# The inverse of the softmax sums: from a reciprocal on VectorE to a logarithm and an exponential on ScalarE with one Newton step, and the order of the work around it

## The chip, the cores and the metric

The kernel runs on one core of a Trainium2 chip. The metric is the device time of one execution in microseconds (us), the median over several runs. PE is TensorE (PEld its loading of weights), DVE is VectorE, ACT is ScalarE, POOL is GpSimd, and SP is the engine that issues most of the DMAs.

## What is computed

Three layers follow each other. The first is attention over hashed buckets (batch 2, 8 heads, 768 positions, 64 features a head):

```
mask = q_bucket[:, :, :, None] == k_bucket[:, :, None, :]
scores = scale * np.matmul(q, k.transpose(0, 1, 3, 2))
scores = np.where(mask, scores, -1000000000.0)
scores = scores - np.max(scores, axis=-1, keepdims=True)
attn = np.exp(scores)
attn = attn / (np.sum(attn, axis=-1, keepdims=True) + 1e-09)
return np.matmul(attn, v)
```

Its result, turned to 1536 tokens of 512 features, goes through a dense layer (a product with w_in, a softmax gate, a layer norm, a product with w_out), and that through a mixture of 8 experts in which each token takes one. The change touches the attention alone: there are 16 (batch, head) pairs, and for each of them 768 sums of exponentials, of which the inverse (with 1e-9 added) scales the 768 columns of the output.

## The kernel before

All engines run programs of their own, written out by hand in the order in which they are to run, and semaphores alone tie them together. The 16 heads go through a software pipeline. In the turn of head h, TensorE does six steps (kt = 0 to 5). Each step holds one block of "leading" scores of a head one or two further on (`leading`, L465, two matmuls of queries in rows; only their maxima are wanted) and the transposed scores of head h against one block of 128 keys (`products`, L481, four matmuls, L491 and L492). ScalarE takes the exponentials of those (`weights_of`, L1022, instruction on L1027) into the tile `PT`, and GpSimd adds them up over the six blocks into `acc` (`add`, L1234, instruction on L1242).

Step kt = 2 of head h holds more: TensorE turns the maxima of head h+1 (`turn_maxima`, L476, instruction on L478), multiplies the second half of the weights of head h-1 with V (`values(h-1, (3, 4, 5))`, twelve matmuls on L503), and adds the sums of head h-1 over the partitions with a matrix of ones (`sums`, L507, four matmuls on L512). After step 5 come `values(h, (0, 1, 2))`, and for even h the hashes of a pair of heads two further on (`hashes`, L455).

VectorE takes the maxima of the leading scores, a block at a time (`maximum`, L727, instruction on L730). The leading scores have two places in PSUM: `leading(h, j)` waits on `s_nm` until maximum j-2 of the same count has been read, so TensorE can be at most two blocks ahead of VectorE. `place_maxima` (L740) writes the turned maxima of the next head into a row of its operand. `inverse` (L748) copies the mean row out of PSUM (L751), adds 1e-9 to the sums (L752) and takes the reciprocal in place (L754) in the tile `rec`; `attended` (L756) forms (values + mean) times `rec` in two instructions (L762) and writes the attention's output `xT`. VectorE's order in the turn of head h is: maxima 4 and 5 of head h+1, the gathering of the six (`maxima`, L732), for odd h the bits of the hashes, maximum 0 of h+2, `place_maxima(h+1)`, `inverse(h-1)`, maximum 1 of h+2, `attended(h-1)`, maxima 2 and 3 of h+2.

ScalarE's order in the turn is: the weights of kt = 0, for odd h the high parts of a later pair, the weights of kt = 1, a scaling of dense-layer weights (L1040), the weights of kt = 2, `weights_high(h)` (L1044), the weights of kt = 3, 4 and 5. GpSimd's order is: for odd h the low parts of a later pair (L1231), the first addition of head h, `weights_low(h)` (L1247), the other four additions.

One PSUM bank, `RB`, holds in turn the maxima turned by TensorE, the sums of a head, and the hashes; another, `PVB`, the products with V. The semaphores `s_mc` (maxima placed), `s_rec` (the steps of the inverse), `s_bits` and `s_fin` (a head's output written) say when they are free. After head 15 the same engines go on with the dense layer: TensorE's `hidden` products (L533 to L535), `soft` on VectorE (from L771) and ScalarE (L1050), the taking of the next tokens (L1057 on ScalarE, L1252 on GpSimd).

Of the kernel before, what the change touches and what calls it, by code (L numbers as in the profile page):

```python
# [39 lines left out]
ACT = mybir.ActivationFunctionType  # L40
# [48 lines left out]
C_SLOT = C_LOW + E * E  # L89
C_TOK = C_SLOT + SLOTS  # L90
C_ALT = C_TOK + NT
C_ALL = C_ALT + E - 1


def constants():

    c = np.zeros((P, C_ALL), np.float32)
    c[:, C_ID:C_ID + P] = np.eye(P)


    for group in range(4):
        for head in range(2):
            for n, sign in enumerate((1, -1) if group % 2 == 0 else (-1, 1)):
                r = slice(group * GROUP + head * BITS + n * NBITS, group * GROUP + head * BITS + (n + 1) * NBITS)
                c[r, C_THR] = LEAST if sign > 0 else -ABOVE
                c[r, C_TOP] = -BIG if group % 2 == 0 else 1.0
                if group < 2:
                    c[:, C_SIGN:C_SIGN + P][:, r] = sign
    c[:, C_TRI:C_TRI + P] = np.triu(np.ones((P, P)), 1)
    c[:, C_ONE:C_ONE + P] = 1  # L110
    c[:, C_EXP:C_EXP + E] = np.arange(E) - E
    c[:, C_J:C_J + NT] = np.arange(NT) * P


    c[:, C_J] = -1
    c[:, C_LOW:C_LOW + E * E] = np.tril(np.ones((E, E)), -1).reshape(1, -1)
    c[:, C_SLOT:C_SLOT + SLOTS] = np.arange(SLOTS)
    for n in range(NT):
        c[:, C_TOK + n] = (n % B) * S + (n // B) * P + np.arange(P)
    c[:, C_ALT:C_ALT + E - 1] = (-1.0) ** np.arange(E - 1)  # L120
    return c


# [11 lines left out]
def build(nc, qT, kT, vP, proj_d, w_solu, g_ln, w_gates, w1, w2, cst_d, out):  # L135
    with ExitStack() as ctx:
# [52 lines left out]
        def many(name, word, n, width, dt=F32):  # L189
            return [at(f"{name}{i}", word + i * width, [P, width], dt)[:, :] for i in range(n)], word + n * width  # L190
# [27 lines left out]
        PT = PT.rearrange("p (k g q) -> p k g q", k=KT, g=2)  # L218
        w = (w + 7) // 8 * 8
        acc, w = many("acc", w, 2, S)  # L220
        (rec,), w = many("rec", w, 1, HALF)
        stg, w = many("stg", w, 2, DM)
        empty = at("empty", mid - 2 * DM, [P, ROW])

# [37 lines left out]
        ld_w = [sem(f"ld_w{c}") for c in range(2)]  # L262
        s_high, s_low, s_ws, s_wh, s_wl = sem("s_high"), sem("s_low"), sem("s_ws"), sem("s_wh"), sem("s_wl")
        ld_v = [sem(f"ld_v{c}") for c in range(2)]
        (s_hash, s_bits, s_slot, s_nm, s_mm, s_mt, s_mc, s_st, s_exp, s_acc, s_pv, s_rb, s_rec,
         s_fin, s_ones, s_zeros) = [sem(n) for n in ("s_hash", "s_bits", "s_slot", "s_nm", "s_mm", "s_mt", "s_mc",
                                            "s_st", "s_exp", "s_acc", "s_pv", "s_rb", "s_rec", "s_fin", "s_ones", "s_zeros")]


        m_xh = sem("m_xh")  # L270
# [24 lines left out]
        def wait(eng, s, v):  # L295

            if not isinstance(v, int) or v > 0:
                eng.wait_ge(s, v)
# [71 lines left out]
        def _(sp):  # L370
# [17 lines left out]
                    fill_2(sp, h, n)  # L388

            def load_v(h):  # L390
                wait(sp, s_rb, h - 1)
                sp.dma_start(V[h % 2], vP[h:h + 1].rearrange("o p (k d) -> p (o k) d", k=KT)).then_inc(ld_v[h % 2], 16)

            def load_w(m):
# [57 lines left out]
        def _(pe):  # L452
# [22 lines left out]

            def turn_maxima(h):  # L476
                pe.wait_ge(s_mm, h + 1)
                m = pe.transpose(PS[0:TILES, RB, 0:P], mm_[:, h % 2 * TILES:(h % 2 + 1) * TILES], ident)  # L478
                m.then_inc(s_mt, 1)

# [26 lines left out]
            def sums(h):  # L507

                pe.wait_ge(s_acc, (KT - 1) * (h + 1))
                wait(pe, s_rec, 3 * h - 1)  # L510
                for g in range(2):
                    m = mm(PS[g * D:(g + 1) * D, RB, 0:HALF], cst[:, C_ONE:C_ONE + D],  # L512
                           acc[h % 2][:, g * HALF:(g + 1) * HALF], start=True, stop=True)
                m.then_inc(s_rb, 1)
# [24 lines left out]
            for h in range(HEADS):  # L539
                for kt in range(KT):  # L540
                    ahead = (h + 1, kt + TILES - 2) if kt < 2 else (h + 2, kt - 2)
                    if ahead[0] < HEADS:
                        leading(*ahead)
                    products(h, kt)
                    if kt == 2:
                        if h + 1 < HEADS:
                            wait(pe, s_rec, 3 * h - 4)
                            pe.wait_ge(s_bits, min(PAIRS, 2 + (h + 1) // 2))
                            turn_maxima(h + 1)
                        if h > 0:  # L550
                            values(h - 1, (3, 4, 5))
                            if h + 1 < HEADS:
                                pe.wait_ge(s_mc, h + 2)
                            sums(h - 1)
                values(h, (0, 1, 2))
                if h % 2 == 0 and h // 2 + 2 < PAIRS:
                    wait(pe, s_rec, 3 * h - 1)
                    hashes(h // 2 + 2, RB)
            hidden(0, 0, 0, True)
            values(HEADS - 1, (3, 4, 5))  # L560
            sums(HEADS - 1)
            hidden(0, 0, 1, True)


# [144 lines left out]
        def _(dve):  # L709
# [17 lines left out]
            def maximum(h, j):  # L727
                col = h % 2 * TILES + j
                dve.wait_ge(s_slot, TILES * h + j + 1)
                dve.tensor_reduce(nm[:, col:col + 1], slot(h, j), AX.XY, ALU.max, negate=True).then_inc(s_nm, 1)  # L730
# [16 lines left out]

            def inverse(h):  # L748

                dve.wait_ge(s_rb, h + 1)  # L750
                dve.tensor_copy(mu[:, h % 2:h % 2 + 1], PS[:, PVB, HALF:HALF + 1]).then_inc(s_rec, 1)  # L751
                dve.tensor_scalar(rec, PS[:, RB, 0:HALF], EPS, None, ALU.add).then_inc(s_rec, 1)  # L752
                dve.wait_ge(s_rec, 3 * h + 2)
                dve.reciprocal(rec, rec).then_inc(s_rec, 1)  # L754

            def attended(h):  # L756

                p, c = h // 2, h % 2
                dve.wait_ge(s_rec, 3 * h + 3)
                for g in range(2):  # L760
                    mine = slice(g * D, (g + 1) * D)
                    m = dve.scalar_tensor_tensor(  # L762
                        out=xT[c * D:(c + 1) * D, p * S + g * HALF:p * S + (g + 1) * HALF], in0=PS[mine, PVB, 0:HALF],
                        scalar=mu[mine, c:c + 1], in1=rec[mine, :], op0=ALU.add, op1=ALU.mult)
                m.then_inc(s_fin, 1)

            def soft(n, b, first):
                h2 = PS[:, 2 * b:2 * b + 2, :]
# [33 lines left out]
            for h in range(HEADS):  # L802
                if h + 1 < HEADS:
                    maximum(h + 1, TILES - 2)
                    maximum(h + 1, TILES - 1)
                    maxima(h + 1)
                if h % 2 == 1 and h // 2 + 2 < PAIRS:
                    hash_bits(h // 2 + 2, RB)
                if h + 2 < HEADS:
                    maximum(h + 2, 0)  # L810
                if h + 1 < HEADS:
                    place_maxima(h + 1)
                if h > 0:
                    inverse(h - 1)
                if h + 2 < HEADS:
                    maximum(h + 2, 1)
                if h > 0:
                    attended(h - 1)
                if h + 2 < HEADS:
                    maximum(h + 2, 2)  # L820
                    maximum(h + 2, 3)
# [194 lines left out]
        def _(act):  # L1016
            fn = nc.scalar.activation

            act.dma_start(hashw[:, :], proj_d).then_inc(s_cst, 16)
            act.dma_start(cst[:, :], cst_d).then_inc(s_cst, 16)  # L1020

            def weights_of(h, kt, g):  # L1022
                act.wait_ge(s_st, 2 * (KT * h + kt) + g + 1)
# [5 lines left out]
            def high_parts(p):  # L1029
                act.wait_ge(ld_r[p % 2], 32 * (p // 2) + 32)  # L1030
                if p > 0:
                    for h in (2 * p - 2, 2 * p - 1):
                        ready_1(act, h)
                        ready_2(act, h)
                for r, high in zip(R[p % 2], (Hq, Hk)):
                    fn(high, r, ACT.Copy).then_inc(s_high, 1)

            def weights_scaled(m):
                act.wait_ge(ld_w[m % 2], 16 * (m // 2) + 16)
# [31 lines left out]
            for h in range(HEADS):  # L1071
                weights_of(h, 0, 0)
                weights_of(h, 0, 1)
                if h % 2 == 1 and h // 2 + 2 < PAIRS:
                    high_parts(h // 2 + 2)
                weights_of(h, 1, 0)
                weights_of(h, 1, 1)
                weights_scaled(h)
                weights_of(h, 2, 0)
                weights_of(h, 2, 1)  # L1080
                if h == HEADS - 1:
                    act.wait_ge(s_rows0, 16 * SLOTS)
                weights_high(h)
                for kt in (3, 4, 5):
                    weights_of(h, kt, 0)
                    weights_of(h, kt, 1)
                if h == HEADS - 2:
                    act.wait_ge(s_fin, HEADS // 2)
                    take(0, 0, 0, True)
            soft(0, 0, True)  # L1090
            act.wait_ge(s_fin, HEADS)
            take(1, 1, 0, True)
# [263 lines left out]
```

## Time and profile before

| | |
|---|---|
| time of the kernel before | 713.75 us, median of 3 runs (712.77 to 714.27) |
| the profiled execution | 709.71 us, its span 707.6 us |
| busy in the span | PE 598.6 us (85%), DVE 400.0 (57%), POOL 268.5 (38%), ACT 259.0 (37%) |
| mean granted clock of TensorE | 0.925 |
| attention | from the start to about 287 us of the span |

The busy time of PE is that of pipelined matmuls, of which the ends are modelled, so its share is not a share of its peak. Shares over the whole span mix the three layers; the attention has to be read by itself, one head's turn at a time. Times in the views are microseconds from the start of the span, unless marked ns.

### The profile page before, as it was taken

To read this page: it belongs to the slowest core of one execution; us is meant where nothing else is said; L and a number is where in the kernel's file an instruction comes from. 1 tells how busy PE (TensorE), PEld (TensorE's weight loads), DVE (VectorE), ACT (ScalarE), POOL (GpSimd) and SP (SyncE) were. 2 spreads that over 40 slices of the span, in tenths; PEclk is the share of its full clock that TensorE was granted. 3 is DMA by queue.
4 is the path that set the end of the run, shared out by engine and by line. 5 is a ranking of instruction groups with operands and counts; after the bars stand their busy time and mean duration, and the time that the engine had idled before them with its cause. 6 is when DMAs were issued, how large, how long until landed. Compare 5 with 4: busy or idle time off the path is not lost.

```text
span 707.6 us, 9729 instructions
## 1 busy us (share of the span) xinstructions
PE 598.6 (85%) x2886; PEld 440.4 (62%) x2887; DVE 400.0 (57%) x525; ACT 259.0 (37%) x403; POOL 268.5 (38%) x188
## 2 busy tenths in 40 slices
PE   3879798888988888699999999602999999999994
PEld 1545454554555544588888887402788788778883
DVE  3737777766677752666566566352445554655611
ACT  1334444444444342122222224312444554545410
POOL 4375767676777675223224223462001010010101
PEclk8689999999999999899999999755999999999997
DMA  6778384674827000300000000347517465665500
GB/s 184 171 215 233 80 239 123 176 192 114 206 69 182 27 12 1 119 1 1 0 0 0 0 0 1 119 157 244 209 51 253 157 213 205 196 217 180 148 19 29
DMA packets 39266, 83.90 MB, mean 119 GB/s; under 512 B 7485, under 2 KB 10429, under 8 KB 39232
## 3 DMA queue, kind: packets, MB, share of 16 engines
q1 hardware_dynamic: 31376, 71.04, 34.5%
q10 hardware_dynamic: 5616, 6.12, 3.4%
q0 software_dynamic: 2240, 6.31, 2.3%
q8 instruction: 18, 0.29, 0.2%
q14 instruction: 16, 0.13, 0.1%
HBM read 52.09 MB, written 12.35 MB: 91 GB/s over the span
## 4 chain that ended last, share of the span: by engine, by line
PE 70%; DVE 13%; issue 4%; DMA 3%; ACT 3%; POOL 2%; SPq 2%; ACTq 1%; DVEq 0%; POOLq 0%
PE PS L503 11%; DVE at_rec L754 6%; PE PS L664 5%; PE PS L666 4%; PE PS L665 4%; PE PS L645 4%; PE PS L646 3%; PE PS L647 3%; PE PS L491 3%; PE PS L533 3%; PE PS L535 3%; PE PS L578 3%; PE PS L534 3%; PE PS L472 3%; PE PS L580 3%
## 5 line engine op out<-in xcount | busy, mean ns | idle before, releaser
L1027 ACT ACTIVATE at_PT<-PS 128x384 f32<-128x384 f32 x192 | 84.6, 491 | 135.2 <-PE PS L492 134.3
L730 DVE TENSOR_REDUCE sb_nm<-PS 128x1 f32<-128x768 f32 x96 | 89.2, 947 | 43.7 <-PE PS L472 41.3
L1242 POOL TENSOR_TENSOR at_acc<-at_acc,at_PT 128x768 f32<-128x768 f32 x64 | 107.6, 1681 | 14.8 <-ACT at_PT L1027 10.3
L952 DVE TENSOR_TENSOR at_W<-at_raw,at_W 128x2048 f32 (+1 forms) x30 | 68.0, 2291 | 71.2 <-ACT at_W L1097 68.5
L1318 POOL DMA_INDIRECT out<-at_yb,sb_to x16 | 15.8, 985 | 204.7 <-DVE at_yb L964 204.7
L1097 ACT ACTIVATE at_W<-at_raw 128x2048 f32 (+1 forms) x32 | 60.4, 1911 | 61.7 <-issue 31.1
L503 PE MATMUL PS<-at_PT,at_V 128*64 128x385 f32 x384 | 80.0, 557 | 3.1 <-DVE at_xT L762 2.7
L472 PE MATMUL PS<-at_B,at_A 76*128 76x384 f32 x192 | 58.6, 394 | 28.0 <-DVE sb_nm L730 23.3
L491 PE MATMUL PS<-at_A,at_B 102*128 102x384 f32 x192 | 73.9, 385 | 9.5 <-ACT at_PT L1027 9.5
L472 PEld LDWEIGHTS PS<-at_B,at_A 76*128 76x128 f32 x192 | 34.4, 205 | 54.9 <-DVE sb_nm L730 31.8
L492 PE MATMUL PS<-at_A,at_B 128*128 128x384 f32 x192 | 67.3, 350 | 0.0
L1273 POOL TENSOR_TENSOR at_cn<-at_eb,sb_mv 128x1024 f32<-128x1024 f32 x12 | 22.7, 1894 | 108.5 <-DVE sb_mv L783 108.5
L664 PE MATMUL PS<-at_W,at_hTh 128*128 x128 | 52.1, 407 | 5.1 <-DVE at_hTl L983 4.9
L645 PE MATMUL PS<-at_W,at_xsh 128*128 x128 | 52.1, 407 | 3.2 <-DVE at_xsl L956 3.2
L503 PEld LDWEIGHTS PS<-at_PT,at_V 128*64 128x64 f32 x384 | 29.1, 152 | 40.4 <-issue 34.4
L491 PEld LDWEIGHTS PS<-at_A,at_B 102*128 102x128 f32 x192 | 37.5, 195 | 26.6 <-ACT at_PT L1027 20.4
L666 PE MATMUL PS<-at_W,at_hTl 128*128 x128 | 50.7, 396 | 0.0
L646 PE MATMUL PS<-at_W,at_xsh 128*128 x128 | 50.5, 395 | 0.0
L665 PE MATMUL PS<-at_W,at_hTh 128*128 x128 | 50.5, 395 | 0.0
L647 PE MATMUL PS<-at_W,at_xsl 128*128 x128 | 50.4, 394 | 0.0
L533 PE MATMUL PS<-at_wsp,at_xch 128*128 128x512 f32 x96 | 39.9, 416 | 6.2 <-POOL at_xcl L1252 6.2
L754 DVE RECIPROCAL at_rec<-at_rec 128x384 f32<-128x384 f32 x16 | 40.9, 2553 | 0.5
(154 smaller groups left out, 1101.6 us busy)
## 6 DMA issues: line engine op xcount, KB each, us to landing
at_raw<-w SPq DMA_DIRECT2D x32, 1024.0 KB, 5.9
at_A<-at_H SPq DMA_DIRECT2D x32, 192.0 KB, 2.7
at_B<-at_H SPq DMA_DIRECT2D x28, 192.0 KB, 3.7
rows_by_expert<-at_empty SPq DMA_DIRECT2D x19, 257.0 KB, 5.3
at_XS<-rows_by_expert ACTq DMA_DIRECT2D x17, 256.0 KB, 2.7
at_stg<-w_solu SPq DMA_DIRECT2D x16, 256.0 KB, 4.0
at_V<-vP SPq DMA_DIRECT2D x16, 192.0 KB, 3.8
at_Re<-qT SPq DMA_DIRECT2D x4, 384.0 KB, 5.0
```

The lines of the kernel that those rows point to most:

```text
L472: m = mm(slot(h, j)[:, g, :], A1[t][0:ROWS1, j * P:(j + 1) * P], B1[t][0:ROWS1, g * HALF:(g + 1) * HALF], start=True, stop=True)
L491: mm(PS[:, STB + g, 0:HALF], B1[t][0:ROWS, at_k], A1[t][0:ROWS, at_g], start=True, stop=False)
L503: m = mm(PS[g * D:(g + 1) * D, PVB, 0:HALF + 1], V[h % 2][:, kt, :], PT[:, kt, g, :], start=(kt == 0), stop=(kt == KT - 1))
L645: mm(PS[:, g, :], xsh[:, x_k], W[:, high], start=(k == 0), stop=False)
L646: mm(PS[:, g, :], xsh[:, x_k], W[:, low], start=False, stop=False)
L664: mm(PS[:, 4 + c, :], hTh[:, h_f], W[:, high], start=(f == 0), stop=False)
L665: mm(PS[:, 4 + c, :], hTh[:, h_f], W[:, low], start=False, stop=False)
L666: m = mm(PS[:, 4 + c, :], hTl[:, h_f], W[:, high], start=False, stop=(f == FB - 1))
L730: dve.tensor_reduce(nm[:, col:col + 1], slot(h, j), AX.XY, ALU.max, negate=True).then_inc(s_nm, 1)
L754: dve.reciprocal(rec, rec).then_inc(s_rec, 1)
L1027: fn(PT[:, kt, g, 0:HALF], PS[:, STB + g, 0:HALF], ACT.Exp, scale=SCALE).then_inc(s_exp, 1)
L1242: pool.tensor_tensor(total, PT[:, 0, :, 0:HALF] if kt == 1 else total, PT[:, kt, :, 0:HALF], ALU.add).then_inc(s_acc, 1)
```

## The change

The reciprocal (L754) and the addition of 1e-9 (L752) leave VectorE. ScalarE takes ln(sum + 1e-9) out of PSUM into `rec`, with 1e-9 as a bias from a new constant column, and then exp(-rec) in place. VectorE refines it by one Newton step in two instructions: err = (sum + 1e-9) times rec, then rec = (2 - err) times rec. ScalarE does its part after `weights_high(h)`.

The order changes as well. TensorE does the sums of head h-1 first, then their products with V, and then turns the maxima of head h+1, now once VectorE has read the sums. VectorE does the inverse and `attended(h-1)` directly after maximum 0 of head h+2, then maximum 1, and `place_maxima(h+1)` only after that. The table set that holds both functions is loaded ahead by name. The load of V waits for the products with V in place of the sums.

```diff
+            act.preload_act_table_set("natural_log_exp_and_others")
...
+            def inverse(h):        # ScalarE
+                act.wait_ge(s_rb, h + 1)
+                wait(act, s_fin, h)
+                fn(rec, PS[:, RB, 0:HALF], ACT.Ln, bias=cst[:, C_EPS:C_EPS + 1]).then_inc(s_ln, 1)
+                act.wait_ge(s_ln, 2 * h + 1)
+                fn(rec, rec, ACT.Exp, scale=-1.0).then_inc(s_ln, 1)
...
             def inverse(h):        # VectorE
-                dve.wait_ge(s_rb, h + 1)
-                dve.tensor_copy(mu[:, h % 2:h % 2 + 1], PS[:, PVB, HALF:HALF + 1]).then_inc(s_rec, 1)
-                dve.tensor_scalar(rec, PS[:, RB, 0:HALF], EPS, None, ALU.add).then_inc(s_rec, 1)
-                dve.wait_ge(s_rec, 3 * h + 2)
-                dve.reciprocal(rec, rec).then_inc(s_rec, 1)
+                dve.wait_ge(s_ln, 2 * h + 2)
+                dve.scalar_tensor_tensor(out=err, in0=PS[:, RB, 0:HALF], scalar=EPS, in1=rec,
+                                         op0=ALU.add, op1=ALU.mult).then_inc(s_rec, 1)
+                dve.wait_ge(s_rec, 4 * h + 1)
+                dve.scalar_tensor_tensor(out=rec, in0=err, scalar=2.0, in1=rec, reverse0=True,
+                                         op0=ALU.subtract, op1=ALU.mult).then_inc(s_rec, 1)
...
             def attended(h):
-                dve.wait_ge(s_rec, 3 * h + 3)
+                dve.wait_ge(s_pv, 2 * h + 2)
+                dve.tensor_copy(mu[:, c:c + 1], PS[:, PVB, HALF:HALF + 1]).then_inc(s_rec, 1)
+                dve.wait_ge(s_rec, 4 * h + 3)
...
             def turn_maxima(h):
                 pe.wait_ge(s_mm, h + 1)
+                wait(pe, s_rec, 4 * (h - 1) - 3)
...
             def sums(h):
                 pe.wait_ge(s_acc, (KT - 1) * (h + 1))
-                wait(pe, s_rec, 3 * h - 1)
+                pe.wait_ge(s_bits, min(PAIRS, 2 + h // 2 + 1))
+                pe.wait_ge(s_mc, min(HEADS, h + 2))
...
                     if kt == 2:        # TensorE
+                        if h > 0:
+                            sums(h - 1)
+                            values(h - 1, (3, 4, 5))
                         if h + 1 < HEADS:
-                            wait(pe, s_rec, 3 * h - 4)
-                            pe.wait_ge(s_bits, min(PAIRS, 2 + (h + 1) // 2))
                             turn_maxima(h + 1)
-                        if h > 0:
-                            values(h - 1, (3, 4, 5))
-                            if h + 1 < HEADS:
-                                pe.wait_ge(s_mc, h + 2)
-                            sums(h - 1)
...
             hidden(0, 0, 0, True)
+            sums(HEADS - 1)
             values(HEADS - 1, (3, 4, 5))
-            sums(HEADS - 1)
             hidden(0, 0, 1, True)
...
                     maximum(h + 2, 0)        # VectorE
+                if h > 0:
+                    inverse(h - 1)
+                    attended(h - 1)
+                if h + 2 < HEADS:
+                    maximum(h + 2, 1)
                 if h + 1 < HEADS:
                     place_maxima(h + 1)
-                if h > 0:
-                    inverse(h - 1)
-                if h + 2 < HEADS:
-                    maximum(h + 2, 1)
-                if h > 0:
-                    attended(h - 1)
```

In the diff the three marks "ScalarE", "VectorE" and "TensorE" are added here to tell which engine's program a piece is in.

## Rows read from the trace of the kernel before

**Rows 1.** Chain that ended last, in the turn of head 8: start, us, engine and line

```profile
161.04 0.67 PE PS L512 x4
...
164.94 0.82 DVE sb_nm L730
```

**Rows 2.** Instructions grouped by line, 50 to 300 us: xcount | busy us, mean ns | idle before

```profile
L1027 ACT ACTIVATE at_PT<-PS 128x384 f32<-128x384 f32 x174 | 76.4, 491 | 126.5 <-PE PS L492 126.0
...
L754 DVE RECIPROCAL at_rec<-at_rec 128x384 f32<-128x384 f32 x16 | 40.9, 2553 | 0.5
...
L762 DVE SCALAR_TENSOR_TENSOR at_xT<-PS,sb_mu,at_rec 64x384 f32<-64x384 f32 x32 | 19.6, 613 | 0.5
...
L1044 ACT ACTIVATE at_wsp<-at_stg 128x512 fp32r<-128x512 f32 x14 | 9.1, 648 | 0.0
L752 DVE TENSOR_SCALAR at_rec<-PS 128x384 f32<-128x384 f32 x16 | 8.8, 548 | 0.0
```

**Rows 3.** Timeline, turn of head 8 (even): start us, us, engine line op [idle before]

```profile
158.68 0.27 PE L478 MATMUL PS<-sb_cst,sb_mm 128*6 128x128 f32 x1
...
159.42 0.64 ACT L1044 ACTIVATE at_wsp<-at_stg 128x512 fp32r<-128x512 f32 x1
...
161.38 1.68 POOL L1242 TENSOR_TENSOR at_acc<-at_acc,at_PT 128x768 f32<-128x768 f32 x1
...
161.73 0.16 DVE L751 COPY sb_mu<-PS 128x1 f32<-128x1 f32 x1 [1.76 <-PE PS L512]
...
163.83 0.34 PE L492 MATMUL PS<-at_A,at_B 128*128 128x384 f32 x1
165.81 0.62 PE L472 MATMUL PS<-at_B,at_A 76*128 76x384 f32 x2 [1.64 <-DVE sb_nm L730]
```

**Rows 4.** Timeline, turn of head 9 (odd): PE and POOL

```profile
176.33 0.27 PE L478 MATMUL PS<-sb_cst,sb_mm 128*6 128x128 f32 x1
...
178.01 1.56 POOL L1242 TENSOR_TENSOR at_acc<-at_PT 128x768 f32<-128x768 f32 x1
179.51 1.32 POOL L1247 TENSOR_TENSOR at_wsp<-at_stg,at_wsp 128x512 fp32r<-128x512 f32 x1
180.76 7.18 POOL L1242 TENSOR_TENSOR at_acc<-at_acc,at_PT 128x768 f32<-128x768 f32 x4
```

**Rows 5.** Line 788: duration ns min/median/max; then the timeline around one such instruction

```profile
L788 DVE TENSOR_TENSOR sb_var_all<-sb_var_all,sb_rs x12: 1758/1764/1772, 292.4 to 438.4; 128x1 f32 x8, 128x1 f32<-128x1 f32 x4
...
306.45 1.76 DVE L788 TENSOR_TENSOR sb_var_all<-sb_var_all,sb_rs 128x1 f32<-128x1 f32 x1
...
306.30 1.89 POOL L1273 TENSOR_TENSOR at_cn<-at_eb,sb_mv 128x1024 f32<-128x1024 f32 x1 [10.92 <-DVE sb_mv L783]
308.14 0.61 POOL L1277 COPY at_x<-at_x2b 128x512 f32<-128x512 f32 x1
```

**Rows 6.** Waits of PE (us in total, times, longest), 52 to 250 us

```profile
PE PS L472 <- DVE sb_nm L730: 21.3, 13, 1.6
```

**Rows 7.** Busy time by stretch: PE, PEld, DVE, ACT, POOL, granted clock, DMA share, GB/s

```profile
150.46:153.87 3.41, 3.41 (x12) 2.04 (x13) 2.61 (x4) 0.98 (x2) 3.12 (x3) 0.50 1.02 303
```

**Rows 8.** Timeline of VectorE: the copy that begins the inverse, turns 5, 6 and 7

```profile
116.02 0.16 DVE L751 COPY sb_mu<-PS 128x1 f32<-128x1 f32 x1 [1.80 <-PE PS L512]
...
130.10 0.16 DVE L751 COPY sb_mu<-PS 128x1 f32<-128x1 f32 x1 [1.76 <-PE PS L512]
...
146.09 0.16 DVE L751 COPY sb_mu<-PS 128x1 f32<-128x1 f32 x1 [1.80 <-PE PS L512]
```

**Rows 9.** Timeline from the end of head 15 into the dense layer

```profile
274.25 2.16 PE L503 MATMUL PS<-at_PT,at_V 128*64 128x385 f32 x12 [1.35 <-DVE at_xT L762]
...
284.69 0.39 PE L535 MATMUL PS<-at_wsp,at_xcl 128*128 128x512 f32 x1
...
286.71 1.23 DVE L771 TENSOR_REDUCE sb_nm<-PS 128x1 f32<-128x1024 f32 x1
```

**Rows 10.** Timeline of ScalarE at the start of the span

```profile
1.70 1.28 ACT L1036 ACT_TABLE_LOAD   x1 [1.54 <-PEq L1349]
```

More of the change, by code:

```diff
@@ L91 @@
 C_ALT = C_TOK + NT
-C_ALL = C_ALT + E - 1
+C_EPS = C_ALT + E - 1
+C_ALL = C_EPS + 1
 def constants():
@@ L120, in constants @@
     c[:, C_ALT:C_ALT + E - 1] = (-1.0) ** np.arange(E - 1)
+    c[:, C_EPS] = EPS
     return c
@@ L220, in build @@
         acc, w = many("acc", w, 2, S)
-        (rec,), w = many("rec", w, 1, HALF)
+        (rec, err), w = many("rec", w, 2, HALF)
         stg, w = many("stg", w, 2, DM)
@@ L264, in build @@
         ld_v = [sem(f"ld_v{c}") for c in range(2)]
-        (s_hash, s_bits, s_slot, s_nm, s_mm, s_mt, s_mc, s_st, s_exp, s_acc, s_pv, s_rb, s_rec,
+        (s_hash, s_bits, s_slot, s_nm, s_mm, s_mt, s_mc, s_st, s_exp, s_acc, s_pv, s_rb, s_ln, s_rec,
          s_fin, s_ones, s_zeros) = [sem(n) for n in ("s_hash", "s_bits", "s_slot", "s_nm", "s_mm", "s_mt", "s_mc",
-                                            "s_st", "s_exp", "s_acc", "s_pv", "s_rb", "s_rec", "s_fin", "s_ones", "s_zeros")]
+                                            "s_st", "s_exp", "s_acc", "s_pv", "s_rb", "s_ln", "s_rec", "s_fin", "s_ones", "s_zeros")]
         m_xh = sem("m_xh")
@@ L390, in load_v @@
             def load_v(h):
-                wait(sp, s_rb, h - 1)
+                wait(sp, s_pv, 2 * h - 2)
                 sp.dma_start(V[h % 2], vP[h:h + 1].rearrange("o p (k d) -> p (o k) d", k=KT)).then_inc(ld_v[h % 2], 16)
@@ L545, in _ @@
                     if kt == 2:
+                        if h > 0:
+                            sums(h - 1)
+                            values(h - 1, (3, 4, 5))
                         if h + 1 < HEADS:
-                            wait(pe, s_rec, 3 * h - 4)
-                            pe.wait_ge(s_bits, min(PAIRS, 2 + (h + 1) // 2))
                             turn_maxima(h + 1)
-                        if h > 0:
-                            values(h - 1, (3, 4, 5))
-                            if h + 1 < HEADS:
-                                pe.wait_ge(s_mc, h + 2)
-                            sums(h - 1)
                 values(h, (0, 1, 2))
                 if h % 2 == 0 and h // 2 + 2 < PAIRS:
-                    wait(pe, s_rec, 3 * h - 1)
+                    pe.wait_ge(s_mc, h + 2)
                     hashes(h // 2 + 2, RB)
             hidden(0, 0, 0, True)
+            sums(HEADS - 1)
             values(HEADS - 1, (3, 4, 5))
-            sums(HEADS - 1)
             hidden(0, 0, 1, True)
@@ L764, in attended @@
                         scalar=mu[mine, c:c + 1], in1=rec[mine, :], op0=ALU.add, op1=ALU.mult)
-                m.then_inc(s_fin, 1)
+                    m.then_inc(s_rec if g == 0 else s_fin, 1)
             def soft(n, b, first):
@@ L1083, in _ @@
                 weights_high(h)
+                if h > 0:
+                    inverse(h - 1)
                 for kt in (3, 4, 5):
@@ L1089, in _ @@
                     take(0, 0, 0, True)
+            inverse(HEADS - 1)
             soft(0, 0, True)
```

## The prediction

> **What bounds the kernel now.** I read the chain of waits first, then the timeline of one even and one odd head. The chain of head 8 leaves TensorE after the sums (161.04 + 0.67) and comes back to it through VectorE, of which the last link is maximum 1 of the head two further on, 164.94 to 165.76 [rows 1]. Between lie the copy, the addition of 0.55 and the reciprocal, 16 of them at 2553 ns [rows 2]. The timeline shows the other side: TensorE has its last product of kt = 4 in hand by 163.83 + 0.34, and then sits idle 1.64 us until 165.81, released by the maximum [rows 3]. So in each turn TensorE waits for VectorE, and VectorE had before that waited 1.76 us for the sums. Whatever shortens the way from sums to maximum 1 is on the path, until TensorE's own work ends later.
>
> I set a mark at the start of the turning of the maxima, 158.68 in head 8 and 176.33 in head 9 [rows 3, 4]. The old order has VectorE start at 3.05 after the mark, the maximum end at 7.08 and TensorE go on at 7.13.
>
> **The change, step by step** (us after the mark; the stretch from the mark to kt = 3 is what is reordered).
>
> TensorE: the sums take 0.67 [rows 1]. Turn, products with V and sums together took until 3.05; without the turn (0.27) they end at 2.78. In the chain the sums begin at 2.36 and VectorE sees them at 3.05, 0.7 later; with 0.2 for the filling of the first matmul ScalarE may start at 0.9.
>
> ScalarE: it is busy with `weights_high` until 159.42 + 0.64, that is 1.38, so that and not the sums lets it begin. The trace holds no logarithm. Nearest are the exponential out of PSUM of the same shape, 491 ns, and a copy in SBUF of 512 columns, 648 ns [rows 2]; both new instructions lie between. I take 0.55 for the first (it has a bias by pointer) and 0.52 for the second, each near the row of its own width: 1.38 + 0.55 + 0.02 + 0.52 = 2.47. ScalarE then idles until the weights of kt = 3, so its 1.1 us a turn cost nothing. Without that cover each would delay the next exponentials.
>
> VectorE, first instruction (err): one operand in PSUM and one in SBUF, as L762 (613 ns) and nearly L752 (548). At 0.61 it ends at 2.50 + 0.61 = 3.11. The removed addition and reciprocal, 3.1 us, go; the copy stays and moves.
>
> VectorE, the Newton step: both tensors in SBUF, 384 columns; I take 0.55, bounds 0.5 to 0.61 by the same two rows. Here stands the question of the whole forecast. The one two-operand SBUF instruction of before that starts while GpSimd computes is L788, on one column: it takes 1758 ns at least, in all 12 cases, and at 306.45 + 1.76 ends as GpSimd's instruction does, 306.30 + 1.89. GpSimd's next, which starts at 308.14, did not hold it up further [rows 5]. I read: such an instruction waits for GpSimd's running one, and then goes first. The Trainium skill, "SBUF — State Buffer", section "Who interferes with whom", gives VectorE's second SBUF port and GpSimd's as one shared pair under an exclusive lock. By that rule the Newton step waits just as L788 does, while by its duration alone it would not; the two sums are those of the first and the third case below.
>
> Even turns: at 3.13 GpSimd is inside an addition from 161.38 for 1.68, until 4.38. The step runs 4.38 to 4.93. The copy adds 0.08, `attended` two times 0.613, maximum 1 takes 0.82: 7.06 to 7.1, and TensorE goes on at 7.13, as before. Gain 0.0 in each of six turns (2 to 12). TensorE still waits there, less long: its turn of the maxima waits for err until 3.13 in place of 2.78, so kt = 3 and 4 end 0.3 later, at 5.8, and the wait is 1.35.
>
> Odd turns: the running addition ends at 178.01 + 1.56 = 179.57, or 3.24, and `weights_low` is next, from 179.51 [rows 4]. The step is ready at 3.13, a tenth earlier, and as L788 goes first: 3.24 + 0.55 + 0.08 + 1.23 + 0.82 = 5.92, TensorE at 5.97 in place of 7.13, or 1.16; it is itself not ready before 5.8. I take 1.1, for seven turns (1 to 13; the first is colder, and taken alike): 7.7.
>
> Turns 14 and 15 have no maximum to wait for; there `values(h, ...)` waits 1.35 for `attended` [rows 9]. That now ends at 4.93 + 0.08 + 1.23 = 6.24, and TensorE is ready at about 6.1 to 6.5. Two times 1.1: 2.2.
>
> After head 15 VectorE's `soft` began at 286.71, right behind `attended`. The half of `hidden` that it needs ends at 284.69 + 0.39 whatever the order before it; now that is last, with `attended` some 2.7 earlier. Gain 1.5.
>
> **The clock.** The 13 waits of TensorE for the maximum sum to 21.3 us [rows 6]. Seven times in the same stretch the granted clock falls to 0.50 for 3.4 us, as at 150.46, right behind this wait in the turn of head 7 [rows 7]: the lower of TensorE's two levels, 1.2 against 2.4 GHz. From copy to copy the turns took 14.08 (from 116.02), 15.99 and, with a fall at 150.46, 15.64 to 161.73 [rows 8, 3]: a turn of the first kind with a fall costs 15.64 less 14.08, 1.56, and one of the other kind 1.6 to 1.7. I take 1.6. In the new order no wait reaches 1.64: odd turns 0.35 and 0.2, even turns 0.35 and 1.35 apart from each other. The trace has no wait of 1.35 by which to tell, so the bounds are all seven falls gone, 11.3, and none, 0. I take all gone, since 6 of the 13 waits of 1.64 already passed without one.
>
> Costed at nothing: the table set (one load of 1.28 us at 1.70, before any input has landed [rows 10], now by name); `place_maxima` about 5 us later, at 7.1 to 8.05, wanted only by the next turn's first products, behind three more steps and the products with V; the load of V, released at 2.9 in place of 3.05 and behind it SP's other loads; GpSimd, held up at most 0.6 a turn by the Newton step, with its run ending 11.6 after the mark in a turn of 15 [rows 4].
>
> Sum: 7.7 + 0 + 2.2 + 1.5 + 11.3 = 22.7 from 709.71, the profiled execution's own time (its span 707.6 and 2.1 around it), which is 687.0. That execution lies 4.0 below the median, so against the median it is **691**.
>
> **The rivals.**
> - The Newton step loses to GpSimd's next instruction in odd turns as well and waits until 179.51 + 1.32 (4.5): all 13 turns gain nothing, 2.2 + 1.5 + 11.3 = 15.0, **699**. For it: the margin is 0.1 us, and errors of 0.1 in three durations of ScalarE and VectorE.
> - It is never held (L788 is a tensor-tensor instruction, this a scalar-tensor-tensor one): 13 times 1.1 + 2.2 + 1.5 + 11.3 = 29.3, **684.5**. Against it: L788, 12 times in 12.
> - The falls stay where 1.35 us of waiting stays: **702** with odd turns free, **710** with all held.
> - Slower: held behind GpSimd's whole run. In odd turns `weights_low` and four additions stand back to back until 180.76 + 7.18, or 11.6. If the step had to wait for an empty engine, maximum 1 would come 11.6 less 3.24 later than at 5.92, 14.3, and TensorE lose 7.1 in each of seven turns: 50 less what the ends give back, **750 to 765**. It decides from about 4.5 on, where the held step makes TensorE later than 7.13. Against it: L788 with another GpSimd instruction right behind.
> - Not done as said: a table load before each logarithm and each exponential, two of 1.28 a turn. The path grows by 2.6 and gains 1.1 at most: 15 times 1.5 or more slower, **735 and up**. For it only that the default choice could differ from the named one.
>
> **How the numbers follow.** The first case has 0.38, held in all turns 0.23, never held 0.12, falls that stay 0.16, the two slower ones 0.05 and 0.03, and 0.03 remains for gains eaten by things that I don't see. The range 682 to 705 takes in the first three cases and the milder of the clock's; without the clock's doubt, the likeliest one's own range is 688 to 695. A measurement of this kernel tells 0.2%, 1.4 us, from no change. Faster by more than that: 0.89; within it 0.03; slower 0.08.
>
> **What would show it.** In the changed profile: the reciprocal's line gone; a logarithm and an exponential of about 0.5 us each, starting 1.3 after the sums' start, one table load at the start; err at 0.6; the Newton step long (1.7 to 1.8) in even turns, ending with GpSimd's addition, and 0.6 to 0.7 in odd ones; turns of about 14.1 and 14.9; waits for the maximum below 1.4; a granted clock of 1.00 between 52 and 230 us. Wrong if the step lasts 1.9 or more in odd turns (699), if it is 0.55 everywhere (684.5), if falls are still there, or if the wait of the maxima's turn is much over 0.4, which would say that ScalarE is later than I take it.

## The result and the profile after

The changed kernel takes 692.14 us (median of 4 runs, 691.57 to 694.88) against 713.26 for the one before: a ratio of 0.974, interval 0.970 to 0.978. The profiled execution took 691.57, its span 689.5. The forecast was 691. The number is close; the clock's term of its sum was not, as the sections below show. One execution of a kernel in the experiments ("Maximum 1 ahead of attended", with the reciprocal: 782.3 us at a mean granted clock of 0.741) is left out of its ratio; without it that kernel's median is 669.0 in place of the 669.2 given there.

First the new instructions, grouped by line (mean ns of one is the last number ahead of the second bar):

```profile
L754 DVE SCALAR_TENSOR_TENSOR at_rec<-at_rec,at_rec 128x384 f32<-128x384 f32 x16 | 21.0, 1313 | 0.6
...
L751 DVE SCALAR_TENSOR_TENSOR at_rec<-PS,at_rec 128x384 f32<-128x384 f32 x16 | 8.9, 557 | 52.2 <-ACT at_rec L1047 52.2
...
L1045 ACT ACTIVATE at_rec<-PS,sb_cst 128x384 f32<-128x384 f32 x15 | 9.0, 598 | 5.5 <-PE PS L516 5.5
L1047 ACT ACTIVATE at_rec<-at_rec 128x384 f32<-128x384 f32 x16 | 8.4, 523 | 0.5
```

The logarithm takes 598 ns, the exponential 523, err (L751) 557, where 0.55, 0.52 and 0.61 had been taken. The Newton step (L754) has the same shape as err but a mean of 1313 ns. Means mix, so the timeline of one even and one odd turn is wanted (heads 8 and 9, start and duration in us; POOL is GpSimd):

```profile
151.75 0.87 PE L516 MATMUL PS<-at_acc,sb_cst 128*64 128x384 f32 x4
...
154.36 1.68 POOL L1256 TENSOR_TENSOR at_acc<-at_acc,at_PT 128x768 f32<-128x768 f32 x1
154.69 1.76 DVE L754 SCALAR_TENSOR_TENSOR at_rec<-at_rec,at_rec 128x384 f32<-128x384 f32 x1
...
158.86 0.62 PE L474 MATMUL PS<-at_B,at_A 76*128 76x384 f32 x2 [1.49 <-DVE sb_nm L730]
...
170.94 1.54 POOL L1256 TENSOR_TENSOR at_acc<-at_PT 128x768 f32<-128x768 f32 x1
...
172.26 0.63 DVE L754 SCALAR_TENSOR_TENSOR at_rec<-at_rec,at_rec 128x384 f32<-128x384 f32 x1
...
172.44 1.61 POOL L1261 TENSOR_TENSOR at_wsp<-at_stg,at_wsp 128x512 fp32r<-128x512 f32 x1
...
175.31 0.62 PE L474 MATMUL PS<-at_B,at_A 76*128 76x384 f32 x2 [0.38 <-DVE sb_nm L730]
```

In the even turn the step starts at 154.69 and ends at 156.45; GpSimd's addition ended at 156.04, so 0.4 us of it came after. TensorE goes on at 158.86, 7.11 after the sums' start, where before it was 7.13 after the mark [rows 3]. In the odd turn (head 9's, from 170.94) the addition ends at 172.48, the step lasts 0.63, and it is now GpSimd's next, `weights_low`, that is drawn out, 1.61 us where it took 1.32 before [rows 4]. TensorE goes on 0.38 us after it was ready.

Not every odd turn is like this one. The step lasts 0.62 to 0.64 in turns 3, 5, 7, 9 and 11, and 1.76 to 1.79 in all even turns and in 13 and 15; in turn 1 it is held by `weights_low`, and after head 15 it takes 0.56. In turn 13 GpSimd has no low parts of a later pair to make, so it is as early as in an even turn, and the step meets its addition:

```profile
50.88 1.34 DVE L754 SCALAR_TENSOR_TENSOR at_rec<-at_rec,at_rec 128x384 f32<-128x384 f32 x1
...
231.35 1.68 POOL L1256 TENSOR_TENSOR at_acc<-at_acc,at_PT 128x768 f32<-128x768 f32 x1
...
231.69 1.77 DVE L754 SCALAR_TENSOR_TENSOR at_rec<-at_rec,at_rec 128x384 f32<-128x384 f32 x1
...
235.87 0.61 PE L474 MATMUL PS<-at_B,at_A 76*128 76x384 f32 x2 [1.51 <-DVE sb_nm L730]
```

The turns' lengths, read from the starts of err in turns 7, 8 and 9 (VectorE's timeline):

```profile
141.10 0.56 DVE L751 SCALAR_TENSOR_TENSOR at_rec<-PS,at_rec 128x384 f32<-128x384 f32 x1 [2.69 <-ACT at_rec L1047]
...
154.10 0.56 DVE L751 SCALAR_TENSOR_TENSOR at_rec<-PS,at_rec 128x384 f32<-128x384 f32 x1 [2.13 <-ACT at_rec L1047]
...
171.67 0.56 DVE L751 SCALAR_TENSOR_TENSOR at_rec<-PS,at_rec 128x384 f32<-128x384 f32 x1 [2.70 <-ACT at_rec L1047]
```

The odd turn's 13.00 us holds its gain, against 14.08 before; the even turn's 17.57 is longer than the 15.99 of before [rows 8]. In it the granted clock has fallen. (Between the starts of `attended` the same two turns, without a fall, take 14.15 and 14.82: the held step moves the mark by 1.1 us, and the sum of the pair is the same 28.97.) TensorE's waits between 52 and 250 us (in total, times, longest), and the first and last of the five stretches in which the clock was low:

```profile
PE PS L474 <- DVE sb_nm L730: 12.7, 13, 1.5
...
PE PS L481 <- DVE at_rec L751: 3.2, 13, 0.3
```

```profile
98.40:101.80 3.40, 3.40 (x12) 1.60 (x12) 2.09 (x3) 0.98 (x2) 2.41 (x2) 0.50 0.64 233
...
221.30:224.70 3.40, 3.40 (x13) 1.24 (x12) 1.55 (x2) 0.65 (x2) 1.84 (x2) 0.50 0.00 0
```

The waits for the maximum fell from 21.3 to 12.7 us [rows 6], but not one of the five turns from an even to an odd head between 90 and 230 us is without a low stretch; they start 30.7 us apart, once in two turns. (Such a stretch of 3.4 us is called a fall below.) Waits of 1.5 us stand in seven turns, the even ones from 2 to 12 and turn 13; behind those of turns 2 and 13 the clock did not fall.

Where the 18.1 us between the two spans were won is read from the marks of turns 1 and 14 (the turning of the maxima before, the sums now) and from VectorE's first two `soft` maxima. The kernel before (the first `soft` maximum, 286.71, is in [rows 9]):

```profile
47.82 0.41 PE L478 MATMUL PS<-sb_cst,sb_mm 128*6 128x128 f32 x1
...
253.62 0.27 PE L478 MATMUL PS<-sb_cst,sb_mm 128*6 128x128 f32 x1
...
300.75 1.23 DVE L771 TENSOR_REDUCE sb_nm<-PS 128x1 f32<-128x1024 f32 x1 [0.49 <-PE PS L535]
```

The changed kernel:

```profile
47.52 1.55 PE L516 MATMUL PS<-at_acc,sb_cst 128*64 128x384 f32 x4
...
242.89 0.87 PE L516 MATMUL PS<-at_acc,sb_cst 128*64 128x384 f32 x4
...
271.78 1.22 DVE L774 TENSOR_REDUCE sb_nm<-PS 128x1 f32<-128x1024 f32 x1 [1.18 <-PE PS L539]
...
284.36 1.22 DVE L774 TENSOR_REDUCE sb_nm<-PS 128x1 f32<-128x1024 f32 x1 [0.46 <-PE PS L539]
```

Ahead of turn 1 lie 0.3 us, in the 13 turns 1 to 13 10.4, from there to `soft` 4.2, and up to the second maximum 1.5, in which the kernel before has one low stretch more. The last 1.7 us come later, 1.6 of them where the kernel before has one more low stretch, at 444 us.

### The profile page after: what moved, and what is told of

It reads as the page before. It is cut to its first block, busy times and chain, and to the rows that moved or that the text cites. A ratio compares the mean times of both kernels' runs of the same rounds, so it can differ in the third digit from the quotient of the medians.

```text
span 689.5 us, 9776 instructions
## 1 busy us (share of the span) xinstructions
PE 590.2 (86%) x2886; PEld 434.5 (63%) x2887; DVE 382.6 (55%) x525; ACT 274.9 (40%) x435; POOL 269.2 (39%) x188
## 4 chain that ended last, share of the span: by engine, by line
PE 62%; DVE 12%; ACT 11%; issue 5%; DMA 4%; POOL 2%; SPq 2%; ACTq 1%; DVEq 0%; POOLq 0%
PE PS L506 6%; PE PS L664 5%; PE PS L666 4%; PE PS L665 4%; PE PS L537 3%; PE PS L645 3%; ACT at_PT L1030 3%; PE PS L539 3%; PE PS L646 3%; PE PS L647 3%; PE PS L538 3%; PE PS L578 3%; PE PS L580 3%; PE PS L579 3%; PE PS L474 3%
## 5 line engine op out<-in xcount | busy, mean ns | idle before, releaser
L506 PE MATMUL PS<-at_PT,at_V 128*64 128x385 f32 x384 | 76.3, 537 | 0.1
L578 PE MATMUL PS<-at_wsp,at_lnh 128*128 128x512 f32 x96 | 38.7, 403 | 1.7 <-DVE at_lnl L838 1.7
```

What stands on the lines that cost most here:

```text
L506: m = mm(PS[g * D:(g + 1) * D, PVB, 0:HALF + 1], V[h % 2][:, kt, :], PT[:, kt, g, :], start=(kt == 0), stop=(kt == KT - 1))
```

## The experiments

All are compared with the kernel before, 713.15 to 713.47 in their series. Two turn lengths given together are the one from an odd to an even head and the one from an even to an odd head, without a fall of the clock.

**The order alone.** The changed kernel's order, with the addition and the reciprocal back on VectorE and nothing of the inverse on ScalarE.

```diff
-                dve.wait_ge(s_ln, 2 * h + 2)
-                dve.scalar_tensor_tensor(out=err, ...)
-                dve.scalar_tensor_tensor(out=rec, in0=err, scalar=2.0, in1=rec, reverse0=True, ...)
+                dve.wait_ge(s_rb, h + 1)
+                wait(dve, s_fin, h)
+                dve.tensor_scalar(rec, PS[:, RB, 0:HALF], EPS, None, ALU.add).then_inc(s_rec, 1)
+                dve.wait_ge(s_rec, 4 * h + 1)
+                dve.reciprocal(rec, rec).then_inc(s_rec, 1)
```

> The new order, with the old addition and reciprocal on VectorE in it and nothing of the inverse on ScalarE. My theory (path terms): after the sums' start VectorE begins at 0.9, reciprocal ends at 4.0, attended 5.3, maximum 6.25, TensorE goes on at 6.3 in place of 7.13: 0.8 in each of 13 turns, 2.4 at turns 14 and 15, 1.5 behind them, and the waits of 0.8 bring no fall of the clock, 8 falls of 1.6 fewer: 686 us, which is less than the changed kernel's 692.1, since the reciprocal has one input in SBUF and is never held by GpSimd. Rival (the new function is what brings the gain): about 713. Rival (both bring a part): 700 to 705.

Measured: 683.2 us, ratio 0.958 (0.954 to 0.962). Faster than the changed kernel, by 9 us, with the slow reciprocal in it. The reciprocal is as long as ever, no wait of TensorE for the maximum reaches 1.2, and over 200 us of attention the mean granted clock is 1.00 (it was 0.96 in the same stretch of the changed kernel):

```profile
PE PS L474 <- DVE sb_nm L730: 14.3, 13, 1.1
...
L754 DVE RECIPROCAL at_rec<-at_rec 128x384 f32<-128x384 f32 x16 | 40.9, 2553 | 0.6
...
50.00:250.00 200.00, 180.15 (x958) 108.19 (x954) 155.50 (x184) 96.41 (x211) 157.07 (x99) 1.00 0.59 149
```

Most of what it has over the changed kernel is the clock: its turns 1 to 13 are 10.7 us shorter together, of which five falls of 1.6 are 8.0. It begins them 1.4 later and loses 3.1 behind them, where two more low stretches stand.

**The function alone.** The old order of all engines, with the new inverse in it.

```diff
                 dve.wait_ge(s_rb, h + 1)
                 dve.tensor_copy(mu[:, h % 2:h % 2 + 1], PS[:, PVB, HALF:HALF + 1]).then_inc(s_rec, 1)
-                dve.tensor_scalar(rec, PS[:, RB, 0:HALF], EPS, None, ALU.add).then_inc(s_rec, 1)
-                dve.reciprocal(rec, rec).then_inc(s_rec, 1)
+                dve.wait_ge(s_ln, 2 * h + 2)
+                dve.scalar_tensor_tensor(out=err, ...).then_inc(s_rec, 1)
                 dve.wait_ge(s_rec, 3 * h + 2)
+                dve.scalar_tensor_tensor(out=rec, in0=err, ...).then_inc(s_rec, 1)
```

> The old order, with the new function. My theory: the sums are seen at 3.05 after the mark as before, the Newton step is ready at 4.85. In even turns GpSimd's pause is at 4.4 to 4.9, so it is done at 5.4 (0.75 gained) or held to 7.1 (1 lost); in odd turns it is held by an addition until 6.2 and ends at 6.75, where the reciprocal ended at 6.26 (0.5 lost). Together with 1.0 at the end and more falls of the clock in odd turns: 709 to 718, no clear gain. Rival (the function is what brings the gain, held or not): 700 or less.

Measured: 698.3 us, ratio 0.980 (0.975 to 0.984). My number was wrong, and the rival's right. Where the step stands was forecast rightly: held in odd turns (3 to 11, 1.73 us each), free in even ones, as the timeline of turns 3 and 4 shows. In turns 1 and 13 it was free as well.

```profile
81.38 5.48 POOL L1259 TENSOR_TENSOR at_acc<-at_acc,at_PT 128x768 f32<-128x768 f32 x3
81.77 1.73 DVE L758 SCALAR_TENSOR_TENSOR at_rec<-at_rec,at_rec 128x384 f32<-128x384 f32 x1
...
95.63 1.68 POOL L1259 TENSOR_TENSOR at_acc<-at_acc,at_PT 128x768 f32<-128x768 f32 x1
97.73 0.56 DVE L758 SCALAR_TENSOR_TENSOR at_rec<-at_rec,at_rec 128x384 f32<-128x384 f32 x1
```

What I had too high was the loss in odd turns (0.3 by the turns' lengths, not 0.5) and the falls, which I expected to grow in number: there are seven low stretches of 3.4 us between 40 and 250 us against nine, and after the first, at 47 us, they all stand behind the five waits of 1.84 of the odd turns. So the function is worth something in the old order too, 15 us by the medians, 11 by the spans of the profiled executions.

**err kept in PSUM.** The changed kernel with err written back over the sums, so that the Newton step has only one input in SBUF. TensorE's turn of the maxima, into the same bank, then waits for the step.

```diff
-                dve.scalar_tensor_tensor(out=err, in0=PS[:, RB, 0:HALF], scalar=EPS, in1=rec, ...)
+                dve.scalar_tensor_tensor(out=PS[:, RB, 0:HALF], in0=PS[:, RB, 0:HALF], scalar=EPS, in1=rec, ...)
...
-                dve.scalar_tensor_tensor(out=rec, in0=err, scalar=2.0, in1=rec, reverse0=True, ...)
+                dve.scalar_tensor_tensor(out=rec, in0=PS[:, RB, 0:HALF], scalar=2.0, in1=rec, reverse0=True, ...)
...
-                wait(pe, s_rec, 4 * (h - 1) - 3)
+                wait(pe, s_rec, 4 * (h - 1) - 2)
```

> The changed kernel, but the product err goes back into the sums' own PSUM bank, so that the Newton step reads one input from SBUF and one from PSUM; the turn of the maxima waits for the Newton step in place of err. My theory (held by GpSimd only with two inputs in SBUF): the step lasts 0.55 to 0.6 in all turns; TensorE waits 1.0 for its turn and is then itself the last, 0.7 gained against before in all 13 turns, 3.2 at the ends, no fall in the turns: 688 us. Rival (held by something else than the second SBUF input, for instance by the wait on its predecessor): step of 1.77 in even turns still, TensorE later by 1.2 for its turn: 698 or more.

Measured: 680.2 us, ratio 0.954 (0.950 to 0.958), better than either forecast. The step takes 557 ns in the mean of all 16, as the group of its line shows; TensorE's waits for the maximum are gone and its turn of the maxima waits 0.8 instead. No fall stands between 53 and 250 us, so five falls of 1.6 are a good part of the 12 us gained on the changed kernel.

```profile
PE PS L481 <- DVE sb_mu L761: 10.9, 13, 0.8
...
L754 DVE SCALAR_TENSOR_TENSOR at_rec<-PS,at_rec 128x384 f32<-128x384 f32 x16 | 8.9, 557 | 0.5
```

That settles the hold: the same step behind the same predecessor, with GpSimd's addition running beside it in even turns as before, is held when both inputs are in SBUF and not when one is in PSUM. That err is here also written to PSUM does not explain it, since behind an err in SBUF the step takes 0.56 too where GpSimd is idle (after head 15, and in the even turns of the function alone).

**Filling TensorE's wait.** The changed kernel with work that computes nothing needed in even turns, where TensorE stands idle.

```diff
                     if ahead[0] < HEADS:
+                        if kt == 5 and h > 0 and h % 2 == 0:
+                            pe.wait_ge(s_fin, h)
+                            for _ in range(6):
+                                pe.transpose(PS[0:TILES, PVB, 0:P], mm_[:, ...], ident)
                         leading(*ahead)
```

The added work runs in turns 2 to 12: in turn 14 no leading scores are left, so nothing is added there.

> The changed kernel with six transposes of 0.11 us added in even turns (2 to 14), into the bank of the products with V once attended has read it, where TensorE otherwise waits about 1.49 us for the maximum. Nothing else moves. My theory (the falls follow a long wait of TensorE): the longest wait in these turns drops to about 0.6, the five falls between 90 and 225 us are gone, 5 times 1.6: 684 us. Rival (the falls have another cause, for instance the pace of the turns itself): 692, falls still there. Rival (the wait counts only where it is above 1.6): not applicable, since it was 1.49 and fell.

Measured: 687.0 us, ratio 0.965 (0.960 to 0.969): 5 us faster for more work. In the timeline of TensorE the wait of 1.49 has become one of 0.52 and one of 0.17, and from 52 to 229 us the clock stays at 1.00:

```profile
154.90 0.82 PE L550 MATMUL PS<-sb_cst,sb_mm 128*6 128x128 f32 x6 [0.52 <-DVE at_xT L770]
155.89 0.61 PE L474 MATMUL PS<-at_B,at_A 76*128 76x384 f32 x2 [0.17 <-DVE sb_nm L735]
```

```profile
52.00:229.00 177.00, 162.17 (x877) 99.04 (x875) 125.06 (x167) 95.62 (x207) 138.62 (x86) 1.00 0.64 166
```

All five falls of the even turns went. One came at 229 us, in turn 13, which has no filler and in which the step is held as well: it stands right behind the one wait of 1.5 us that was left.

```profile
227.94 0.62 PE L474 MATMUL PS<-at_B,at_A 76*128 76x384 f32 x2 [1.50 <-DVE sb_nm L735]
...
229.30:232.70 3.40, 3.40 (x12) 1.04 (x12) 1.42 (x2) 0.51 (x2) 1.71 (x2) 0.50 0.00 0
```

From `attended` to `attended` an even turn took 14.82 here and 16.45 in the changed kernel: 1.63 for one fall, with the same path through VectorE.

**Maximum 1 ahead of attended.** If only the way from the sums to TensorE's awaited block counts, `attended` need not stand on it. This edit was put into three kernels: into the order alone (with the reciprocal), into the changed kernel, and into the one with err in PSUM, there with the turn of the maxima after the products of kt = 3.

```diff
                 if h > 0:
                     inverse(h - 1)
-                    attended(h - 1)
                 if h + 2 < HEADS:
                     maximum(h + 2, 1)
+                if h > 0:
+                    attended(h - 1)
```

In the third kernel, besides:

```diff
-                        if h + 1 < HEADS:
-                            turn_maxima(h + 1)
+                    if kt == 3 and h + 1 < HEADS:
+                        turn_maxima(h + 1)
```

> The new order with the old addition and reciprocal on VectorE (as in the run order_only), and in it maximum 1 of head h+2 between the inverse and attended, as it stood in the old kernel. My theory (from the sums to TensorE's awaited block only inverse and maximum 1 need to stand): the reciprocal ends 4.1 after the sums' start, maximum 1 at 5.0, TensorE is itself ready at 5.35 and waits no more; the 13 waits of 1.11 of order_only go, 14.4: 683.2 less 14.4 is 669 us. Rival (attended, now 1 us later, holds the products with V): 675 or more. Rival (only the new function lets the inverse off the path): not below 680.

> The changed kernel with one edit, maximum 1 of head h+2 between the inverse and attended. My theory: even turns, with the Newton step held as before, go on 1.4 earlier, odd ones 0.35 earlier, both to where TensorE itself is ready, and the five falls of the clock go (1.6 each): 8.4 + 2.5 + 8.2 from 692.1, 673 us. Rival (the hold by GpSimd costs more than these waits show): 680 or more.

> As the run err_in_psum (err in the sums' own bank), with maximum 1 between inverse and attended, and with TensorE turning the maxima after the products of kt = 3 in place of before them. My theory: the wait of TensorE for its turn (0.84 in each of 13 turns) goes, 10.9 from 680.2: 669 us, the same as with the reciprocal, since TensorE sets the end in both. Rival (ScalarE's and VectorE's shorter inverse is worth something still): 665 or less. Rival (place_maxima comes too late): 675 or more.

Measured: 669.2 us, ratio 0.937 (0.934 to 0.939), with the reciprocal; 674.0, ratio 0.946 (0.944 to 0.948), for the changed kernel; 666.4, ratio 0.935 (0.933 to 0.936), with err in PSUM. The first and the third are not told apart by their intervals. Their turns are the same, 12.22 / 14.03 and 12.22 / 14.01 from `attended` to `attended`, though the one has a reciprocal of 2553 ns in the inverse and the other takes ScalarE and VectorE 2.2 us together. The second's are longer, 13.43 / 13.76: its TensorE still waits 0.25 us a turn for err, which is half of it. The waits of TensorE in the kernel with the reciprocal, between 52 and 225 us, hold nothing of VectorE any more:

```profile
PE PS L494 <- ACT at_PT L1030: 5.0, 8, 0.9
```

and its timeline shows how little of the inverse is left to wait for, since it runs under the products with V (141.82 to 143.93) and the step behind them:

```profile
141.12 0.87 PE L516 MATMUL PS<-at_acc,sb_cst 128*64 128x384 f32 x4
...
142.63 2.55 DVE L754 RECIPROCAL at_rec<-at_rec 128x384 f32<-128x384 f32 x1
...
145.10 0.90 DVE L730 TENSOR_REDUCE sb_nm<-PS 128x1 f32<-128x768 f32 x1
...
146.25 0.51 PE L474 MATMUL PS<-at_B,at_A 76*128 76x384 f32 x2
```

**ScalarE a little later.** The changed kernel with one more copy in front of each logarithm.

```diff
+                fn(err, cst[:, 0:HALF], ACT.Copy)
                 fn(rec, PS[:, RB, 0:HALF], ACT.Ln, bias=cst[:, C_EPS:C_EPS + 1]).then_inc(s_ln, 1)
```

> The changed kernel with one more copy of 384 columns on ScalarE in front of each logarithm, about 0.45 us. My theory (the Newton step gets in between two GpSimd instructions in odd turns by 0.2 us, and else waits for the next one): in odd turns the step comes too late for that and lasts 1.6 to 1.8 in place of 0.63, so these seven turns lose about 1.3 each and get long waits too; even turns keep their time, since the step was held past that anyway: 692.1 plus 9, with up to 6 more falls of the clock: 701 to 711. Rival (no hold, a mere delay): 0.45 in all 13 turns, 698.

Measured: 695.4 us, ratio 0.977 (0.974 to 0.979). In odd turns the step now starts inside `weights_low` and is held by it (head 9's turn):

```profile
173.07 1.28 POOL L1262 TENSOR_TENSOR at_wsp<-at_stg,at_wsp 128x512 fp32r<-128x512 f32 x1
173.31 1.47 DVE L754 SCALAR_TENSOR_TENSOR at_rec<-at_rec,at_rec 128x384 f32<-128x384 f32 x1
...
174.32 7.48 POOL L1257 TENSOR_TENSOR at_acc<-at_acc,at_PT 128x768 f32<-128x768 f32 x4
```

Two turns without a fall last 14.14 + 16.06 = 30.20, against 14.15 + 14.82 = 28.97 where none fell in the changed kernel's order: 1.23 lost a pair, about the 1.3 foreseen. But the time is lower than foreseen, since the falls went: one between 52 and 250 us, where I expected more. (Behind the turns it lost 3.0 us, with two more low stretches there.) The longest wait for the maximum was 1.2 here, the rest having moved to the turn of the maxima (0.7).

## Why the prediction came out, step by step

**The path, and the new order on it.** Right in its sum, and in most turns. In odd turns 14.08 less 13.00 is 1.08, for 1.1 taken; in even turns 0.0 for 0.0 (TensorE at 7.11 for 7.13). There two errors cancel: the held step ended 4.70 after the mark for 4.93, and the copy, `attended` and the maximum behind it took 2.36 for 2.13. The sum booked 1.1 for each of seven odd turns. Turns 3 to 11 gave about 1.06 each, 5.3; turn 13, in which the step was held, gave nothing; turn 1 gave 3.4, of which one fall is 1.6. With 0.2 from the even turns that is 7.2 for the 7.7 booked. Turns 14 and 15 and the way to `soft` gave 4.2 for 3.7. TensorE's own work was ready at 5.62 for the 5.8 taken, since err came a little earlier and its turn of the maxima waited 0.25 us for 0.35. In the runs with maximum 1 ahead, where that work alone sets the turn, it is what bounds.

**The Newton step.** Right but for turns 1 and 13, and it was what the forecast hung on. Held in even turns (1.76 to 1.78), free in odd turns 3 to 11 (0.62 to 0.64): the likeliest case. That turn 13, without low parts on GpSimd, would go as an even turn was not seen. That the cause is the second input in SBUF beside GpSimd is shown by the run with err in PSUM. In the odd turns the step starts 0.2 us ahead of the end of GpSimd's addition, and the run with a later ScalarE shows that with 0.4 us more it misses that place. The rule of the Trainium skill, "SBUF — State Buffer", section "Who interferes with whom", of one shared pair of ports under an exclusive lock, agrees with these runs, and with GpSimd's `weights_low` drawn out from 1.32 to 1.61 us. In no run was the step held by more than one GpSimd instruction; the rival in which it waits for the whole run of additions (750 to 765) did not come about, even in the run with a later ScalarE, where `weights_low` has four additions right behind it, or in the function alone, where the step went behind the first of three.

**The clock.** Here the step "I take all gone" failed. The wait in even turns was 1.49, not 1.35: VectorE was done when foreseen (7.06), TensorE ready 0.2 earlier. Behind it the clock still fell, five times from 90 to 230 us. I had refused to draw a line between 1.35 and 1.64 and then chosen the side that I liked; the range held both. In the turns seven became five, 3.2 us at the 1.6 of the term, where it had 11.3. The mean granted clock, 0.925 over 707.6 us and 0.935 over 689.5, says that about 17 us of low clock went in the whole span, five stretches of 3.4. The three besides were in no term: one at 45 us, ahead of turn 1, where no more than 0.3 was won in all, one at 290 us (1.5) and one at 444 (1.6).

**The sum.** Against its own execution the forecast was 687.0 and the measurement 691.6. The path brought 7.2 + 4.2 = 11.4, just what its terms add up to; the clock's term is too high by 8.1 in the turns, and the falls behind the attention gave 3.0 that were not in the sum; the remaining 0.5 lies ahead of turn 1 and at the end. Against the median the forecast was 691 and the measurement 692.1, so near by luck: the profiled execution of the old kernel was 3.6 below its median, and that of the new one 0.6. The old kernel's executions lie between 709.1 and 715.5. What makes this spread is open, and the mean clock does not tell it: the fastest of them (709.07 us) has 0.924, the slowest (715.53) 0.930, and two executions of the changed kernel at 0.935 and 0.947 took 691.57 and 691.73. So a low stretch is priced here by the turns and stretches of work in which one stands, not by the mean clock.

**Costed at nothing.** The attention has one table load, at 1.70 for 1.28 us as before. `place_maxima` and the load of V had no one waiting for them.

**What the change is worth by its parts.** Order alone 30 us, function alone 15, both 21. The function, put into the new order, costs 9 us, as it brings an instruction that GpSimd holds and, behind that, the falls. With maximum 1 ahead of `attended` it still costs 5 (674.0 against 669.2). Nothing of the new function is needed: with the sums ahead of the products with V the reciprocal runs beside TensorE's work, and with maximum 1 in its old place ahead of `attended` it is off the path altogether (669.2 us).

## What to carry to other kernels

Before a slow instruction is replaced, ask whether its inputs can come earlier: a reciprocal of 2.55 us, run beside TensorE's products and with nothing else of VectorE between it and the awaited maximum, cost nothing, and a replacement less than half as long was held by a neighbour. Count for each new VectorE instruction how many of its inputs lie in SBUF, and look at what GpSimd is doing at that moment; one input moved to PSUM was worth 12 us here, falls of the clock among them. Where waits of TensorE are shortened, do not book the clock's share before it is known behind which waits it falls, and break up the longest wait first.

## What the runs showed of the hardware that was not expected

A scalar-tensor-tensor of 128 x 384 with two inputs in SBUF took 557 to 560 ns beside an idle GpSimd and up to 1.79 us beside a busy one, ending 0.4 us after GpSimd's running instruction and ahead of its next. In the turns from 54 us on the granted clock fell to 0.50 behind 7 of the 13 waits of 1.64 us of TensorE in the kernel before, 5 of the 7 of 1.5 in the changed kernel and 5 of the 5 of 1.84 in the function alone. It hardly ever fell where the longest wait was 1.2 or less: never in the order alone, once in the kernel with the later ScalarE, never in the four in which no wait in the turns reaches 0.9. Why some of the waits of 1.5 and 1.64 passed without a fall was not shown. Useless transposes of 0.8 us in such a wait made the kernel 5 us faster.
